# Query transposes by halves of 64 tokens, one burst for each pair of heads

## The reference

```python
def reference(**kwargs):
    attn_out = _attn_ref(q, k, v)                  # (8, 8, 576, 64)
    x = attn_out.transpose(0, 2, 1, 3).reshape(B * S, H * D)      # (4608, 512)
    x = _moe_ref(x, w_in, w_out)                   # 512 -> 2048 -> 512, relu squared
    return _moe2_ref(x, w_gate, w_val, w_out, rms_g)   # rms norm, silu gate, 512 -> 1536 -> 512

def _attn_ref(q, k, v):                            # linear attention
    q_s = np.exp(q - np.max(q, axis=-1, keepdims=True))
    q_s = q_s / (np.sum(q_s, axis=-1, keepdims=True) + 1e-09)
    k_s = np.exp(k - np.max(k, axis=2, keepdims=True))
    k_s = k_s / (np.sum(k_s, axis=2, keepdims=True) + 1e-09)
    kv = np.einsum('bhsd,bhse->bhde', k_s, v)
    return np.einsum('bhsd,bhde->bhse', q_s, kv)
```

## Time and profile before

| | us |
|---|---|
| median of 3 runs | 1665.97 (1665.57 to 1666.49) |
| the profiled execution, its own time | 1665.29 |
| its span, first to last instruction | 1663.5 |
| TensorE busy | 1643.8 (99%) |
| VectorE busy | 1156.9 (70%) |
| ScalarE busy | 616.7 (37%) |
| GpSimd busy | 595.7 (36%) |

### The profile page before, as it was taken

How to read it: one execution, slowest core, us unless ns; L and a number is a source line. 1 busy time by engine, 2 the same in 40 slices (tenths; PEclk the granted TensorE clock), 3 DMA queues, 4 the chain that set the end, 5 groups by cost and what they waited for, 6 DMA issues and landing times.

```text
span 1663.5 us, 27042 instructions
## 1 busy us (share of the span) xinstructions
PE 1643.8 (99%) x10246; PEld 1496.7 (90%) x10246; DVE 1156.9 (70%) x1749; ACT 616.7 (37%) x1056; POOL 595.7 (36%) x470
## 2 busy tenths in 40 slices
PE   7999999999999999999999999999999998999999
PEld 6999999999988888888888989988988988999999
DVE  6687667666667778888766565546556568877775
ACT  5544334433323333333333333333333344334332
POOL 3554324332002225432237644555555552000000
PEclk9999999999999999999999999999999999999999
DMA  7675545554552353344342323232331244434441
GB/s 262 201 242 182 176 157 191 182 170 145 202 176 89 120 173 120 119 123 125 118 142 70 109 88 134 70 134 75 108 102 63 99 143 163 145 121 149 153 137 54
DMA packets 151745, 230.10 MB, mean 138 GB/s; under 512 B 11840, under 2 KB 75840, under 8 KB 151616
## 3 DMA queue, kind: packets, MB, share of 16 engines
q1 hardware_dynamic: 151616, 228.38, 41.5%
HBM read 143.39 MB, written 84.93 MB: 137 GB/s over the span
## 4 chain that ended last, share of the span: by engine, by line
PE 93%; POOL 2%; DVE 2%; issue 1%; ACT 1%; DMA 0%; SPq 0%; DVEq 0%; POOLq 0%; ACTq 0%
PE bank L1819 16%; PE bank L1820 16%; PE bank L1821 16%; PE bank L1905 7%; PE bank L1906 7%; PE bank L1907 7%; PE bank L1995 5%; PE bank L1996 5%; PE bank L1997 5%; PE bank L1812 2%; PE bank L1792 1%; PE bank L1808 1%; PE bank L1840 1%; PE bank L1841 1%; PE bank L1842 1%
## 5 line engine op out<-in xcount | busy, mean ns | idle before, releaser
L1819 PE MATMUL bank<-TR,SW 128*128 128x512 f32 (+1 forms) x840 | 308.5, 367 | 0.3 <-DVE TR L1554 0.3
L1821 PE MATMUL bank<-TR,SW 128*128 128x512 f32 (+1 forms) x840 | 308.7, 368 | 0.0
L1820 PE MATMUL bank<-TR,SW 128*128 128x512 f32 (+1 forms) x840 | 308.6, 367 | 0.0
L1819 PE MATMUL bank<-TAR,SA 128*128 128x288 f32 x784 | 249.1, 318 | 0.1
L1820 PE MATMUL bank<-TAR,SA 128*128 128x288 f32 x784 | 231.2, 295 | 0.0
L1821 PE MATMUL bank<-TAR,SA 128*128 128x288 f32 x784 | 230.4, 294 | 0.0
L1905 PE MATMUL bank<-GH,W 128*128 128x512 f32 x576 | 224.2, 389 | 0.4 <-DVE GH L1459 0.4
L1906 PE MATMUL bank<-GH,W 128*128 128x512 f32 x576 | 224.2, 389 | 0.0
L1907 PE MATMUL bank<-GH,W 128*128 128x512 f32 x576 | 224.2, 389 | 0.0
L1145 ACT ACTIVATE GH<-g 128x512 fp32r<-128x512 f32 x144 | 91.1, 634 | 241.6 <-DVE g L1454 161.6
L1995 PE MATMUL bank<-SW,OA 128*128 128x256 f32 x630 | 179.0, 284 | 0.0
(11 more groups left out here) (176 smaller groups left out, 3309.4 us busy)
## 6 DMA issues: line engine op xcount, KB each, us to landing
h_scratch<-hb SPq DMA_DIRECT2D x128, 288.0 KB, 2.6
hst<-h_scratch SPq DMA_DIRECT2D x144, 256.0 KB, 2.7
araw<-a_scratch SPq DMA_DIRECT2D x18, 1536.0 KB, 6.8
a_scratch<-group SPq DMA_DIRECT2D x72, 256.0 KB, 2.0
xst<-xn_scratch SPq DMA_DIRECT2D x10, 1024.0 KB, 5.1
xn_scratch<-x SPq DMA_DIRECT2D x9, 1024.0 KB, 5.4
a_scratch<-group SPq DMA_DIRECT2D x48, 192.0 KB, 1.9
out<-ost SPq DMA_DIRECT2D x36, 256.0 KB, 2.1
```

Source lines behind the costliest of these rows:

```text
L1819: nc.tensor.matmul(ps[:, 0:w], w_hi[:, cc], x_hi[:, c], start=opens and c == 0, stop=False, skip_group_check=True)
L1820: nc.tensor.matmul(ps[:, 0:w], w_lo[:, cc], x_hi[:, c], start=False, stop=False, skip_group_check=True)
L1821: last = nc.tensor.matmul(ps[:, 0:w], w_hi[:, cc], x_lo[:, c], start=False, stop=c == 1, skip_group_check=True)
```

## The change

In batches 1 to 7 the rounds Q0 and Q1 are done in one place, after the product of the base's step, by a new function `turn_queries`. Each transpose takes 64 tokens: those in the lower half of the partitions go to the bank of Q0 ("even"), those in the upper half to the bank of Q1 ("odd"). There are nine transposes in place of five (nine halves of 64 tokens hold the 576). Both banks are waited for ahead of the first. ScalarE then copies 320 and 256 columns, in blocks of 64 at every other place of `qT`, in place of 384 and 192; the copy of Q1 moves a step forward. The X rounds wait for both copies. Batch 0 stays as it was.

```diff
-UNIT_PE = [("KM", -3), ("Q0", 0), ("Q1", 1), ("KV", 2), ("X0", 6), ("X1", 7)]
+UNIT_PE = [("KM", -3), ("Q", 0), ("KV", 2), ("X0", 6), ("X1", 7)]
-UNIT_ACT = [("qexp", -7), ("kexp", -1), ("readQ0", 1), ("readQ1", 2), ("readX0", 7), ("readX1", 8)]
+UNIT_ACT = [("qexp", -7), ("kexp", -1), ("readQ0", 1), ("readQ1", 1), ("readX0", 7), ("readX1", 8)]
...
+                    if b == 0:
...
+                    else:
+                        blocks = m.qT.rearrange("p (n t) -> p n t", t=D)[:, half::2]
+                        nc.scalar.activation(blocks, ps[:, 0:(SJ - half) * D].rearrange("p (n t) -> p n t", t=D), ACT.Copy)\
+                          .then_inc(taken_act, 1)
...
-                    wait_taken(pe, ROUND_NO[b, "Q1" if half else "Q0", c] - 1)
+                    wait_taken(pe, ROUND_NO[b, "Q1" if half or b else "Q0", c] - 1)
...
+            def turn_queries(b, c):
+
+                n = ROUND_NO[b, "Q0", c]
+                even, odd = round_bank(n - 1), round_bank(n)
+                wait_bank(pe, n - 1)
+                wait_bank(pe, n)
+                q = bufs(b, c).q.rearrange("p j h d -> p j (h d)")
+                pe.wait_ge(q_norm, unit(b, c))
+                for j in [FULL] + list(range(FULL)):
+                    first = nc.tensor.transpose(even[:, j * D:(j + 1) * D], q[0:D, j], ident[0:D, 0:D])
+                    if j == FULL - 1:
+                        first.then_inc(rnd_ready, 1)
+                    if j < FULL:
+                        second = nc.tensor.transpose(odd[:, j * D:(j + 1) * D], q[D:P, j], ident[D:P, D:P])
+                        if j == FULL - 1:
+                            second.then_inc(rnd_ready, 1)
```

More of the change, by code:

```diff
@@ L91 @@
 ROUND_KINDS = ("K0", "K1", "KV", "KM", "Q0", "Q1", "X0", "X1")
+PAIRED = {"Q": ("Q0", "Q1")}
 def alone_tasks(kinds, others=()):
@@ L168 @@
 ROUNDS = [(0, what, c) for _, what, c in ALONE_PE if what in ROUND_KINDS]
-ROUNDS += [(b, what, c) for at in sorted(PE_AT) for what, b, c in PE_AT[at]]
+ROUNDS += [(b, kind, c) for at in sorted(PE_AT) for what, b, c in PE_AT[at] for kind in PAIRED.get(what, (what,))]
 ROUND_NO = {r: n + 1 for n, r in enumerate(ROUNDS)}
@@ L1096, in take_round @@
                 elif kind[0] == "Q":
-                    cols = slice(0, Q_CUT * P) if half == 0 else slice(Q_CUT * P, S)
-                    nc.scalar.activation(m.qT[:, cols], ps[:, 0:cols.stop - cols.start], ACT.Copy).then_inc(taken_act, 1)
+                    if b == 0:
+                        cols = slice(0, Q_CUT * P) if half == 0 else slice(Q_CUT * P, S)
+                        nc.scalar.activation(m.qT[:, cols], ps[:, 0:cols.stop - cols.start], ACT.Copy).then_inc(taken_act, 1)
+                    else:
+                        blocks = m.qT.rearrange("p (n t) -> p n t", t=D)[:, half::2]
+                        nc.scalar.activation(blocks, ps[:, 0:(SJ - half) * D].rearrange("p (n t) -> p n t", t=D), ACT.Copy)\
+                          .then_inc(taken_act, 1)
                 else:
@@ L2011, in _ @@
                 for what, b, c in PE_AT.get(n, []):
-                    do_round(what, b, c)
+                    if what == "Q":
+                        turn_queries(b, c)
+                    else:
+                        do_round(what, b, c)
             for q in range(PA, NQA):
```

## The result

The changed kernel takes 1670.20 us (median of 18 runs), the kernel before 1665.46 (18 runs): +4.7 us, a ratio of 1.0028 (95% interval 1.0022 to 1.0034). The forecast was +5.1 us, 0.31%.

The account below looks back on a forecast made before the run. TensorE was taken as the bound, so 2.8 us for the bursts and 2.3 us for the stalls gave +5.1 us on the median 1665.97: 1671.1 us, 0.31% slower. The range was 1666.5 to 1677.8 us.

Parts of the forecast that it names:

- The bound: TensorE, busy 330.39 of 331 us where the change works; a nanosecond more or less there is one in the end.
- The burst: A unit's nine half transposes in one place: 0.637 us against 0.538 before, +2.8 us over 28 units.
- The slot: Time for one pair of half transposes on TensorE, taken from KV: 0.0575 us, five of them 0.288.
- the way in and out: Going into halves on TensorE and out again, paid once for each burst: 0.349 us, read from KV.
- a change of rows alone empties the array: Batch 0's KV goes from `128*64` to `64*64` with the same 0.15 us gap, so switching rows alone drains TensorE.
- Halves side by side: In the burst, upper halves run beside lower ones, with pairs 0.0575 us apart; 0.11 would show turns.
- The rival in which they take turns: Loads or halves alternate in the burst: 0.87 to 0.90 us each, 1677.5 to 1678.4 us in all; chance 0.14.
- The wait for KM's bank: In c0 units of batches 2 to 7 the burst waits for VectorE's KM read: 5 x 0.43 + 0.18 = +2.3 us.
- A sign: In c0 units of batches 2 to 7, first load 0.06 us after KM's read, idle time put down to VectorE's line.
- Costless: ScalarE's copies (576 columns in all), the DMA reloading the queries, and KV (0.92 us) were to add no time.

Follow-up runs that it names:

- The two kernels without the wait: The changed kernel with the c0 burst of batches 2 to 7 a step later (1668.46 us), or with KM and its read a step earlier there (1667.94 us).
- the half last block: The kernel before, with only the last block of a unit (64 tokens) transposed as 64 rows: 1673.64 us, +8.3 us.
- the lower-half kernel: The changed kernel, with the four upper transposes reading the lower halves again, so all nine use the same rows: 1676.95 us, +11.6 us over before.
- the kernel with whole transposes: The changed kernel without halves: five whole transposes in one place, both banks waited for first, old copies of 384 and 192 columns: 1669.08 us, +3.4 us over before.

## Why the prediction was right

- **The bound.** Right: 4.67 us more at the end of the first stage, 4.7 in the medians.
- **The burst.** Forecast 0.637, measured 0.649. The slot is 0.062 rather than 0.0575, five of them 0.31; the way in and out is 0.34, as read from KV (0.349). Over what Q0 and Q1 cost in finer times (0.329 + 0.214) it is +0.106, 28 times +3.0 us (forecast +2.8). The two kernels without the wait give +2.7 and +2.6.
- **That a change of rows alone empties the array.** Read from one gap of 0.15 us inside batch 0's KV; shown by the half last block, 8.3 us for nothing but a shape.
- **Halves side by side.** Was open in the prediction; shown by the lower-half kernel. The rival in which they take turns would have been 0.893 a burst.
- **The wait for KM's bank.** Forecast 2.3 us. In the trace the c0 bursts cost 0.900 (batch 2) and 1.089 to 1.096 (3 to 7); over 0.649 that is 0.25 and five times 0.44, 2.46 in all. Per unit that is the 0.43 forecast. But not all of it is added, since some bursts waited before the change too: batch 2's c0 unit 0.10 for the queries (Q0 cost 0.429 there), its c1 unit 0.21 for KM's bank (0.06 now), and batch 1's c0 unit 1.02 for the queries (0.86 now). A TensorE that arrives later waits less there. Net the waits of the bursts grew by 2.0 us.
- **The two parts don't add up exactly.** The wait alone costs 3.4 us, the halves alone 2.6 to 2.7, both together 4.7. In a c0 unit of the kernel with whole transposes the wait costs 1.15 - 0.55 = 0.60, in the changed one 0.44: halves couldn't have begun before the array was empty anyway, at 0.22 in place of 0.13 after the last matmul, so 0.09 of the wait is free. The prediction had that (0.43 for the change, 0.52 for a burst without the emptying). The rest of the 0.16 lies in the first starts of the burst after a wait: the second half starts 0.08 after the first in place of 0.11, the second whole transpose 0.14 after the first in place of 0.11.
- **Missed.** X0 of batch 2's first unit had a wait of its own before the change: it and the KM behind it cost 1.30 us, and 1.04 after. The stall ahead of it hides 0.25 us of that wait, which is back in the two kernels without the stall (1.29 and 1.22), so by the traces these should be 2.2 to 2.3 us under the change, and they are 2.0 to 2.1 under it; the prediction named no such gain. A sign was missed as well: the idle time ahead of the bursts was to be put down to VectorE's line, and the profile puts most of it down to "issue".
- **The sum as the traces have it.** 3.0 for the bursts, 2.0 for the waits added, less 0.25 at X0, makes 4.7, which is what was measured. The forecast of 5.1 had the first term 0.2 too low, the second 0.3 too high, and lacked the third; it is near by its mechanism, and a little by terms that offset each other.
- **Costless.** Copies, DMAs and KV behaved as said: KV 0.929 against 0.927. With two bursts and the copies put a step later KV did wait, so that cover is less than a step.

No kernel here beats the one before. The remedy for the stall brings the change only to +2.6 us; what remains is the switch.

## What to carry to other kernels

Before cutting a matmul into row or column tiles in the middle of whole-array work, price the way in and out, 0.34 us here for either kind of tile, against what the tiles save; five transposes of 0.108 us are too few (by 0.34 / (0.1086 - 0.062) = 7.3 it would take eight, worked out and not tried), and splitting one burst into two, or slipping in a single half, costs that again. Where two steps are put in one place, the buffers of both are needed at the earlier time: look up who frees the second one, and when. And read a cost first in something like it that the kernel already does: KV's 20 matmuls gave the price of a shape that had never run in it.

## What was not expected of the hardware

TensorE did not keep the program's order between transposes in different halves of the rows. With all five lower halves first, the first upper one started 0.12 us after the first lower one, ahead of three lower ones, and the burst took 0.705 us, not the 0.893 of nine in one half. Within a half each transpose started about 0.06 us or more after the one before; whether their order was the program's can't be told from the trace, but for the last of each half, which the program has last too (it is the one that raises the semaphore). How far such overtaking reaches, and whether it holds for other matmuls than these, was not tried.

Idle time ahead of the bursts was put down to "issue" in the profile, 2.0 of 2.3 us, though what ended it was VectorE's read, 0.07 us before. The kernels with the burst later and KM earlier show who it was.
